# Three PSUM bank pairs kept out of one block's second matmul round, with the output accumulator cleared later

## The chip, the cores and the metric

The kernel runs on one core of one Trainium2 chip. The metric is the device time in microseconds of one launch. Of the kernel before, three runs took 655.49, 655.88 and 656.5 us; the median is 655.88 us.

## What is computed

The reference has three parts, run one after the other on 1152 tokens of 512 features (2 batches of 576 tokens, 8 heads of 64).

1. Attention: for each batch and head, a pooled attention over 144 means of four tokens, repeated four times, plus a local attention in a band of width 7.
2. A layer `g = elu(x @ w_in)`, `y = g @ w_out`, with 2048 hidden features.
3. Four gated experts: `h = max(y @ w1[e], 0)`, `out += p[:, e] * (h @ w2[e])`, with 1024 hidden features each and `p` normalised over the experts.

All is in float32. The kernel splits each matmul operand in two float32r parts, hi and lo, and adds three products (hi hi, hi lo, lo hi), so each product is three matmuls.

## The kernel before, in words

The code is written out engine by engine: each engine has its own list of instructions, and semaphores order them. Nothing is planned by a tool; what stands in the list is the order.

The stages are: the attention of batch 0 alone; four blocks of layer 2 on batch 0, mixed with the attention of batch 1; one block of layer 2 on batch 1 (`group1`); three blocks of layer 2 on the same batch in another form (`block7`, w = 5, 6, 7, called here the first, second and third block); then sixteen steps of the experts (`step2`, `down2`). A block is one slice of 512 hidden features. `block7` and `step2` compute the first product by seven half-size products in place of eight, which are put together by sums on DVE.

A `block7` on TensorE (PE) has two rounds. In the up round it makes seven products for each of two column pairs p = 0, 1, in three pairs of PSUM banks: A = (0, 3), B = (1, 4), C = (2, 5). DVE forms sums over them, ACT takes the exponential of the elu, DVE its maximum (`max_part`) and the lo part (`lo_part`). In the down round (`down(g, f)`) it multiplies the hidden features by `w_out`, in eight groups g = 0 to 7. Each group is 12 matmuls of 288 columns into the bank `DOWN7_BANKS[g]`. Groups 0 to 3 are made in two passes, six matmuls of each and then the other six of each; groups 4 to 7 are made one after the other. DVE adds each finished group to `y_acc` (line 1352) and then runs `beside(g)`, some other work written there:

- first block: `token_sums(g)`, which for g = 0 to 3 makes one of four sums of the other half of the tokens (`add_y`, lines 1432 to 1443);
- second block: `gates(g)`, small operations on the gate;
- third block: `nothing(g)`.

Each addition to `y_acc` raises the semaphore `y_added`. PE waits on it before it writes a bank again. `y_before` is its value when all groups of the block before have been added. In the kernel before, the eight groups of a block have eight different banks, so no group waits for an addition of its own block; the waits stand ahead of the first products of the next block.

Between the second and the third block DVE waits until POOL has made the lo parts of all weight sums (`s_lo_ready`, line 1638), whose raw form lies in the space of `o_acc`, and then sets `o_acc` to zero (line 1553). The third block's DVE work, first `sum_u2` (line 1301), stands behind that. `sum_c22` (line 1311) comes after `sum_u2`, `sum_w`, two `max_part` and two `lo_part`; PE waits for it ahead of the last seven-product pair of bank B (the first matmul of line 572 with `t_hi` and `wa_hi`). POOL makes lo parts of weights and tokens all the while; ACT makes the hi parts.

After the third block DVE forms four sums for the experts (`add_y(1, n)`) and PE goes on with `step2(0, 0)`.

Of the kernel before, what the change touches and what calls it, by code (L numbers as in the profile page):

```python
# [13 lines left out]
BATCH, HEADS, SEQ, HD = 2, 8, 576, 64  # L14
# [29 lines left out]
KC = DM // 128  # L44
FB = 512
FC = FB // 128
BLOCKS1 = D_FF // FB
HALVES2 = D_FF2 // FB
N1 = HALF
T1 = SEQ // N1  # L50
# [4 lines left out]

BLOCKS7 = 3
FIRST7 = 2 * BLOCKS1 - BLOCKS7
DOWN7_BANKS = (6, 7, 0, 3, 1, 4, 2, 5)
XT_COLS = slice(256, 256 + N1)

QF = FB // 2
# [26 lines left out]
OUT_CREDIT, Y_CREDIT, DOWN2_CREDIT, UNIT_CREDIT = 2, len(MOE_BANKS), len(DOWN2_BANKS), PAIRS2  # L88
# [18 lines left out]
def program(nc, q, k, v, w_in, w_out, probs, w1, w2, out):  # L107
# [12 lines left out]
    with ExitStack() as ctx:  # L120
        def sb(name, shape, dt=F32):
            return ctx.enter_context(nc.sbuf_tensor(name, shape, dt))

        def sem(name):
            return ctx.enter_context(nc.semaphore(name))
# [7 lines left out]
        o_acc = sb("o_acc", [128, MT, DM])  # L133
# [82 lines left out]
        def xt_at(t):  # L216

            if t == T3_:
                return slice(None), slice(0, 2), slice(SEQ + N1, 2 * SEQ)
            return slice(None), t, slice(None), XT_COLS  # L220
# [13 lines left out]
        zeros_set, pad_set, acc_zeroed = sem("zeros_set"), sem("pad_set"), sem("acc_zeroed")  # L234
# [10 lines left out]
        s_raw_ready, s_hi_ready, s_lo_ready = sem("s_raw_ready"), sem("s_hi_ready"), sem("s_lo_ready")  # L245
# [15 lines left out]
        y_added = sem("y_added")  # L261
# [25 lines left out]

        GROUPS_LAYER1 = GROUPS1 * BLOCKS1 * BATCH
        UPS_LAYER1 = UP1 * BLOCKS1 * BATCH
        YS_LAYER1 = Y_CREDIT + T1 * KC * BLOCKS1 * BATCH  # L290


        @block.sync
# [82 lines left out]
        def _(pe):  # L376
# [192 lines left out]
            def product2(bank, w_op, x_op, start, stop, done):  # L569

                for k in range(2):
                    nc.tensor.matmul(bank, w_op[0][:, k, :], x_op[0][:, k, :], start=(start and k == 0), stop=False,  # L572
                                     skip_group_check=True)
                    nc.tensor.matmul(bank, w_op[0][:, k, :], x_op[1][:, k, :], start=False, stop=False,  # L574
                                     skip_group_check=True)
                    last = nc.tensor.matmul(bank, w_op[1][:, k, :], x_op[0][:, k, :], start=False, stop=(stop and k == 1),  # L576
                                            skip_group_check=True)
                last.then_inc(done, 1)

            def block7(w):  # L580

                v = w - FIRST7
                t0 = SEQ
                y_before = Y_CREDIT + T1 * KC * w
                h_before = UP1 * w

                def weights(fh, kh, p):
                    at = (slice(None), slice(2 * kh, 2 * kh + 2), slice(QF * fh + 128 * p, QF * fh + 128 * (p + 1)))
                    return wa_hi[at], wa_lo[at]

                def weight_sum(n, p):
                    at = (slice(None), n, slice(None), slice(128 * p, 128 * (p + 1)))
                    return s_hi[at], s_lo[at]

                def tokens(kh, th):
                    at = (slice(None), slice(2 * kh, 2 * kh + 2), slice(t0 + N1 * th, t0 + N1 * (th + 1)))
                    return x_hi[at], x_lo[at]

                def token_sum(n):
                    return t_hi[xt_at(n)], t_lo[xt_at(n)]  # L600

                def bank(banks, p):
                    return psum[:, banks[p], 0:N1]

                pe.wait_ge(wa_lo_ready, KC * w + 2)
                for p in range(PAIRS2):
                    pe.wait_ge(y_added, y_before - 5 + p)
                    product2(bank(BANK_A, p), weights(0, 0, p), tokens(0, 0), True, False, p1_done)
                pe.wait_ge(xt_lo_ready, 1)
                pe.wait_ge(s_lo_ready, 3 * v + 1)  # L610
                for p in range(PAIRS2):
                    pe.wait_ge(y_added, y_before - 3 + p)
                    product2(bank(BANK_B, p), weight_sum(S2, p), token_sum(T2_), True, False, p6_done)
                pe.wait_ge(wa_lo_ready, KC * (w + 1))
                for p in range(PAIRS2):
                    pe.wait_ge(p1_copied, PAIRS2 * v + p + 1)
                    product2(bank(BANK_A, p), weights(0, 1, p), tokens(1, 0), False, True, p2_done)
                pe.wait_ge(xt_lo_ready, 2)
                pe.wait_ge(s_lo_ready, 3 * v + 2)
                for p in range(PAIRS2):  # L620
                    pe.wait_ge(y_added, y_before - 1 + p)
                    product2(bank(BANK_C, p), weight_sum(S1, p), token_sum(T1_), True, False, p5_done)
                pe.wait_ge(xt_lo_ready, 4)
                for p in range(PAIRS2):
                    pe.wait_ge(u2_ready, PAIRS2 * v + p + 1)
                    product2(bank(BANK_B, p), weights(1, 0, p), tokens(0, 1), False, False, p7_done)
                for p in range(PAIRS2):
                    pe.wait_ge(c22_ready, PAIRS2 * v + p + 1)
                    product2(bank(BANK_B, p), weights(1, 1, p), token_sum(T4_), False, True, p4_done)
                pe.wait_ge(s_lo_ready, 3 * v + 3)  # L630
                for p in range(PAIRS2):
                    pe.wait_ge(w_ready, PAIRS2 * v + p + 1)
                    product2(bank(BANK_C, p), weight_sum(S4, p), tokens(1, 1), False, True, p3_done)

                def down(g, f):

                    tt, c = divmod(g, KC)
                    t, cols = slice(t0 + N1 * tt, t0 + N1 * (tt + 1)), slice(128 * c, 128 * (c + 1))
                    to = psum[:, DOWN7_BANKS[g], 0:N1]
                    nc.tensor.matmul(to, wb_hi[:, f, cols], h_hi[:, f, t], start=(f == 0), stop=False)  # L640
                    nc.tensor.matmul(to, wb_hi[:, f, cols], h_lo[:, f, t], start=False, stop=False)  # L641
                    last = nc.tensor.matmul(to, wb_lo[:, f, cols], h_hi[:, f, t], start=False, stop=(f == FC - 1))  # L642
                    if f == FC - 1:
                        last.then_inc(group_done, 1)

                pe.wait_ge(wb_lo_ready, FC * (w + 1))
                pe.wait_ge(h_lo_ready, h_before + 2)
                for g in range(KC):
                    if g >= 2:
                        pe.wait_ge(h_lo_ready, h_before + g + 1)  # L650
                    down(g, 0)
                    down(g, 1)
                for g in range(KC):
                    if g == 0:
                        pe.wait_ge(h_lo_ready, h_before + 5)
                    down(g, 2)
                    if g == 0:
                        pe.wait_ge(h_lo_ready, h_before + 6)
                    down(g, 3)
                pe.wait_ge(h_lo_ready, h_before + 8)  # L660
                for g in range(KC, 2 * KC):
                    for f in range(FC):
                        down(g, f)

            def step2(j, b):
# [26 lines left out]
                    pe.wait_ge(h_lo_ready, UPS_LAYER1 + TILES_STEP * (v - 1) + PAIRS2 * place + p + 1)  # L692

                if isinstance(j, int) and v == 0:
                    pe.wait_ge(y_added, YS_LAYER1 - 4)
                pe.wait_ge(y_lo_ready, Y_PARTS * b + 2)
                pe.wait_ge(wa_lo_ready, KC * w + 2)
                for p in range(PAIRS2):
# [2 lines left out]
                pe.wait_ge(y_lo_ready, Y_PARTS * b + 3)  # L701
                pe.wait_ge(s_lo_ready, 3 * (j + BLOCKS7) + 1)
                for p in range(PAIRS2):
                    pe.wait_ge(y_added, YS_LAYER1 - 3 + p)
                    bank_free(3, p)
                    product2(bank(BANK_B, p), weight_sum(S2, p), token_sum(T2_), True, False, p6_done)
                pe.wait_ge(y_lo_ready, Y_PARTS * b + 6)
# [3 lines left out]
                    product2(bank(BANK_A, p), weights(0, 1, p), tokens(1, 0), False, True, p2_done)  # L711
                pe.wait_ge(s_lo_ready, 3 * (j + BLOCKS7) + 2)
                for p in range(PAIRS2):
                    pe.wait_ge(y_added, YS_LAYER1 - 1 + p)
                    bank_free(2, p)
                    product2(bank(BANK_C, p), weight_sum(S1, p), token_sum(T1_), True, False, p5_done)
                for p in range(PAIRS2):
# [106 lines left out]
            with pe.Fori(FIRST7, 2 * BLOCKS1) as w:  # L824
                block7(w)
# [325 lines left out]
        def _(dve):  # L1151
# [127 lines left out]
            def block7(w, beside):  # L1279
# [68 lines left out]
                for g in range(2 * KC):  # L1348
                    tt, c = divmod(g, KC)
                    at = (slice(None), c, slice(t0 + N1 * tt, t0 + N1 * (tt + 1)))  # L1350
                    dve.wait_ge(group_done, groups_before7(w) + g + 1)
                    nc.vector.tensor_tensor(y_acc[at], psum[:, DOWN7_BANKS[g], 0:N1], y_acc[at], ALU.add).then_inc(y_added, 1)
                    beside(g)
# [195 lines left out]

            block7(FIRST7 + 1, gates)  # L1550

            dve.wait_ge(s_lo_ready, 3 * BLOCKS7)
            nc.vector.memset(o_acc[:], 0.0).then_inc(acc_zeroed, 1)

            def nothing(g):
                pass

            block7(FIRST7 + 2, nothing)
            dve.wait_ge(gate_step, 4)
            for n in range(4):  # L1560
                add_y(1, n)
# [187 lines left out]
```

## Time and profile before

| | |
|---|---|
| median of 3 runs | 655.88 us |
| the profiled execution's own time | 655.88 us |
| its span, first to last instruction | 654.0 us |
| PE busy | 643.4 us (98%) |
| DVE busy | 346.9 us (53%) |
| ACT busy | 287.2 us (44%) |
| POOL busy | 324.4 us (50%) |
| mean granted TensorE clock | 0.999 |

The busy time of PE is that of its matmuls, whose ends are modelled and overlap; the distance from one start to the next is the better measure of its pace. PEld is the load of the weights, which runs beside the matmuls. An engine's idle time costs something only if the engine that sets the end waits for it. A line number in a row is that of the instruction in the listing above; a helper's line serves all its callers.

### The profile page before, as it was taken

What the parts mean: (1) busy time and instruction counts of PE and PEld (TensorE: products, weight loads), DVE (VectorE), ACT (ScalarE), POOL (GpSimd) and SP (SyncE); (2) the same over time, 40 slices, a digit from 0 to 9 for tenths busy, and PEclk for the clock granted to TensorE, in tenths of its full rate; (3) what the DMA queues carried; (4) which work ended last, traced back from release to release, by engine and by line L of the source; (5) the groups of instructions that cost most, each with busy time, mean ns of one, the idle gap of its engine ahead of it and who ended that gap; (6) DMA issues with size and microseconds to landing.
All of it is one profiled execution on the core that took longest, in us unless ns stands there. A gap on an engine that the chain in (4) does not pass through costs nothing.

```text
span 654.0 us, 12954 instructions
## 1 busy us (share of the span) xinstructions
PE 643.4 (98%) x4698; PEld 592.7 (91%) x4698; DVE 346.9 (53%) x758; ACT 287.2 (44%) x778; POOL 324.4 (50%) x282
## 2 busy tenths in 40 slices
PE   8999999999999999999999999999999999999998
PEld 5788999999999999998998898899899899899986
DVE  5856454545456876675544544453464355365342
ACT  4878383838295685564223133142162152142210
POOL 4674444344388799898326237137056065160200
PEclk9999999999999999999999999999999999999999
DMA  9854333322112132301203003002011012010012
GB/s 180 229 140 124 106 99 102 102 70 97 64 66 79 64 117 64 114 15 66 66 1 128 1 0 128 0 29 100 0 64 64 0 64 64 2 64 1 2 49 96
DMA packets 51491, 46.13 MB, mean 71 GB/s; under 512 B 31616, under 2 KB 33920, under 8 KB 51456
## 3 DMA queue, kind: packets, MB, share of 16 engines
q1 hardware_dynamic: 51456, 45.67, 23.6%
q8 instruction: 21, 0.34, 0.2%
q14 instruction: 14, 0.11, 0.1%
HBM read 43.30 MB, written 2.36 MB: 70 GB/s over the span
## 4 chain that ended last, share of the span: by engine, by line
PE 86%; SPq 4%; ACT 4%; DVE 2%; issue 2%; DMA 1%; POOL 0%; ACTq 0%; POOLq 0%; DVEq 0%
PE psum L499 15%; PE psum L500 15%; PE psum L501 15%; PE psum L572 11%; PE psum L576 10%; PE psum L574 10%; SPq L298 2%; PE psum L642 2%; PE psum L641 2%; PE psum L640 2%; DMA k_in<-in_k 1%; SPq L309 1%; ACT attn L852 1%; PE psum L491 1%; DVE neg_max L1188 1%
## 5 line engine op out<-in xcount | busy, mean ns | idle before, releaser
L1597 POOL TENSOR_TENSOR wb_lo<-wb_raw,wb_hi 128x512 fp32r<-128x512 f32 x64 | 81.6, 1292 | 185.5 <-ACT wb_hi L886 185.5
L1412 DVE SCALAR_TENSOR_TENSOR o_acc<-psum,gate_now,o_acc 128x512 f32<-128x512 f32 x72 | 54.1, 751 | 126.0 <-PE psum L501 125.7
L501 PE MATMUL psum<-wb_hi,h_lo 128*128 128x512 f32 x288 | 112.3, 390 | 0.0
L500 PE MATMUL psum<-wb_lo,h_hi 128*128 128x512 f32 x288 | 112.2, 390 | 0.0
L499 PE MATMUL psum<-wb_hi,h_hi 128*128 128x512 f32 x288 | 112.0, 389 | 0.0
L996 ACT ACTIVATE h_hi<-psum 128x320 fp32r<-128x320 f32 (+1 forms) x128 | 52.5, 412 | 87.3 <-DVE psum L1384 40.3
L1597 POOL TENSOR_TENSOR wa_lo<-wa_raw,wa_hi 128x512 fp32r<-128x512 f32 x60 | 77.5, 1316 | 17.4 <-ACT wa_hi L927 17.4
L1002 ACT COPY sums<-psum 128x256 f32<-128x256 f32 (+1 forms) x32 | 12.8, 400 | 155.1 <-PE psum L576 155.1
L576 PE MATMUL psum<-x_hi,wa_lo 128*128 128x256 f32 (+2 forms) x228 | 67.4, 296 | 0.0
L574 PE MATMUL psum<-x_lo,wa_hi 128*128 128x256 f32 (+2 forms) x228 | 67.3, 295 | 0.0
L572 PE MATMUL psum<-x_hi,wa_hi 128*128 128x256 f32 (+2 forms) x228 | 67.3, 295 | 0.0
L501 PEld LDWEIGHTS psum<-wb_hi,h_lo 128*128 128x128 f32 x288 | 54.1, 188 | 11.3
L499 PEld LDWEIGHTS psum<-wb_hi,h_hi 128*128 128x128 f32 x288 | 54.1, 188 | 10.9
L1366 DVE SCALAR_TENSOR_TENSOR h_lo<-psum,h_hi 128x320 fp32r<-128x320 f32 (+1 forms) x128 | 54.8, 450 | 17.1 <-ACT h_hi L996 17.0
L500 PEld LDWEIGHTS psum<-wb_lo,h_hi 128*128 128x128 f32 x288 | 54.0, 188 | 10.8
L499 PE MATMUL psum<-h_hi,wb_hi 128*128 128x288 f32 x160 | 48.5, 303 | 0.0
L501 PE MATMUL psum<-h_hi,wb_lo 128*128 128x288 f32 x160 | 47.1, 294 | 0.0
L500 PE MATMUL psum<-h_lo,wb_hi 128*128 128x288 f32 x160 | 47.1, 294 | 0.0
L574 PE MATMUL psum<-t_lo,s_hi 128*128 128x320 f32 (+2 forms) x152 | 44.9, 295 | 0.0
L576 PE MATMUL psum<-t_hi,s_lo 128*128 128x320 f32 (+2 forms) x152 | 44.8, 295 | 0.0
L572 PE MATMUL psum<-t_hi,s_hi 128*128 128x320 f32 (+2 forms) x152 | 44.8, 295 | 0.0
L572 PEld LDWEIGHTS psum<-x_hi,wa_hi 128*128 128x128 f32 x228 | 43.0, 189 | 0.6
(193 smaller groups left out, 1682.9 us busy)
## 6 DMA issues: line engine op xcount, KB each, us to landing
wa_raw<-in_moe_w_in SPq DMA_DIRECT2D x8, 1024.0 KB, 5.3
wb_raw<-in_moe_w_out SPq DMA_DIRECT2D x8, 1024.0 KB, 5.0
wa_raw<-in_moe_w SPq DMA_DIRECT2D x8, 1024.0 KB, 5.0
wb_raw<-in_moe_w SPq DMA_DIRECT2D x8, 1024.0 KB, 5.0
out<-o_acc SPq DMA_DIRECT2D x9, 256.0 KB, 2.0
q_in<-in_q SPq DMA_DIRECT2D x10, 144.0 KB, 5.0
k_in<-in_k SPq DMA_DIRECT2D x10, 144.0 KB, 4.8
v_in<-in_v SPq DMA_DIRECT2D x5, 288.0 KB
```

The source lines that it names most:

```text
L298: sp.dma_start(dst[:, :, HD * h:HD * (h + 1)], src[:, :, h, :]).then_inc(loaded[held(u)], 16)
L499: nc.tensor.matmul(bank_cols, w_hi(n), x_hi_(n), start=(n == 0), stop=False)
L500: nc.tensor.matmul(bank_cols, w_hi(n), x_lo_(n), start=False, stop=False)
L501: last = nc.tensor.matmul(bank_cols, w_lo(n), x_hi_(n), start=False, stop=(n == chunks - 1))
L572: nc.tensor.matmul(bank, w_op[0][:, k, :], x_op[0][:, k, :], start=(start and k == 0), stop=False, skip_group_check=True)
L574: nc.tensor.matmul(bank, w_op[0][:, k, :], x_op[1][:, k, :], start=False, stop=False, skip_group_check=True)
L576: last = nc.tensor.matmul(bank, w_op[1][:, k, :], x_op[0][:, k, :], start=False, stop=(stop and k == 1), skip_group_check=True)
L640: nc.tensor.matmul(to, wb_hi[:, f, cols], h_hi[:, f, t], start=(f == 0), stop=False)
L996: nc.scalar.activation(h_hi[:, 2 * fh + p, t0 + width * th:t0 + width * (th + 1)], psum[:, bank[p], 0:width], ACT.Relu).then_inc(h_hi_read ...
L1366: nc.vector.scalar_tensor_tensor(h_lo[at], bank(banks, p), 0.0, h_hi[at].bitcast(F32), ALU.max, ALU.subtract).then_inc(h_lo_ready, 1)
L1412: nc.vector.scalar_tensor_tensor(o_acc[:, m, :], psum[:, DOWN2_BANKS[(MT * half + m) % 2], :], gate_now[:, m:m + 1], o_acc[:, m, :], ALU.m ...
L1597: nc.gpsimd.tensor_tensor(lo[:, c, :], raw[:, c, :], hi[:, c, :].bitcast(F32), ALU.subtract).then_inc(lo_ready, 1)
```

## The change

The down groups 4 to 7 of each `block7` no longer use banks 1, 4, 2 and 5. They take banks 6, 7, 6 and 7 again, which groups 0 and 1 used. So PE waits ahead of each of them until the group that last used the bank has been added: group 4 for group 0, 5 for 1, 6 for 4, 7 for 5. Groups 0 and 1 get the wait for the block before, and the up round waits less (only p = 1 of B and C; this is needed after the `group1` block). `step2` loses its four waits on `y_added` inside and gets one. The clearing of `o_acc`, with its wait, moves from between the second and third block to `beside(0)` of the third block, behind the addition of group 0.

```diff
-DOWN7_BANKS = (6, 7, 0, 3, 1, 4, 2, 5)
+DOWN7_BANKS = (6, 7, 0, 3, 6, 7, 6, 7)
...
# block7, product of bank pair B (weight sum S2)
                 for p in range(PAIRS2):
-                    pe.wait_ge(y_added, y_before - 3 + p)
+                    if p == 1:
+                        pe.wait_ge(y_added, y_before - 3)
...
# block7, product of bank pair C (weight sum S1)
                 for p in range(PAIRS2):
-                    pe.wait_ge(y_added, y_before - 1 + p)
+                    if p == 1:
+                        pe.wait_ge(y_added, y_before - 2)
...
# block7, down round
                 for g in range(KC):
-                    if g >= 2:
+                    if g < 2:
+                        pe.wait_ge(y_added, y_before - 1 + g)
+                    else:
                         pe.wait_ge(h_lo_ready, h_before + g + 1)
                     down(g, 0)
                     down(g, 1)
...
                 for g in range(KC, 2 * KC):
+                    pe.wait_ge(y_added, y_before + (1, 2, 5, 6)[g - KC])
                     for f in range(FC):
                         down(g, f)
...
# step2, bank pairs B and C
-                    pe.wait_ge(y_added, YS_LAYER1 - 3 + p)
+                    if p == 1:
+                        pe.wait_ge(y_added, Y_CREDIT + T1 * KC * BLOCKS1 * BATCH)
...
-                    pe.wait_ge(y_added, YS_LAYER1 - 1 + p)
...
# DVE
-            dve.wait_ge(s_lo_ready, 3 * BLOCKS7)
-            nc.vector.memset(o_acc[:], 0.0).then_inc(acc_zeroed, 1)
-
-            def nothing(g):
-                pass
-
-            block7(FIRST7 + 2, nothing)
+            def clear_out(g):
+                if g == 0:
+                    dve.wait_ge(s_lo_ready, 3 * BLOCKS7)
+                    nc.vector.memset(o_acc[:], 0.0).then_inc(acc_zeroed, 1)
+
+            block7(FIRST7 + 2, clear_out)
```

## Rows read from the trace of the kernel before

**Rows 1.** Engines and granted clock, from the page: busy us (share), instructions; then 40 slices.

```profile
PE 643.4 (98%) x4698; PEld 592.7 (91%) x4698; DVE 346.9 (53%) x758; ACT 287.2 (44%) x778; POOL 324.4 (50%) x282
...
PEclk9999999999999999999999999999999999999999
```

**Rows 2.** Busy time by engine in the three blocks: stretch, its length, then each engine.

```profile
core 0: us, PE busy (x) PEld busy (x) DVE busy (x) ACT busy (x) POOL busy (x), PEclk, DMA share, GB/s
202.92:227.02 24.10, 24.10 (x182) 23.87 (x181) 19.80 (x40) 16.99 (x40) 18.66 (x14) 1.00 0.18 58
227.02:251.11 24.09, 24.09 (x183) 23.86 (x181) 15.04 (x38) 17.30 (x41) 23.93 (x20) 1.00 0.28 90
251.11:276.12 25.01, 24.11 (x183) 23.87 (x182) 17.31 (x35) 15.34 (x37) 24.39 (x20) 1.00 0.25 84
```

**Rows 3.** Timeline of PE at the wait for `sum_c22`, blocks one and three: start, duration.

```profile
210.71 0.29 PE L576 MATMUL psum<-x_hi,wa_lo 128*128 128x288 f32 x1
211.00 0.40 PE L572 MATMUL psum<-t_hi,wa_hi 128*128 128x288 f32 x1
211.24 0.29 PE L574 MATMUL psum<-t_lo,wa_hi 128*128 128x288 f32 x1
...
258.89 0.29 PE L576 MATMUL psum<-x_hi,wa_lo 128*128 128x288 f32 x1
260.09 0.40 PE L572 MATMUL psum<-t_hi,wa_hi 128*128 128x288 f32 x1 [0.90 <-DVE psum L1311]
```

**Rows 4.** Timeline of DVE at the same two places (x2: two instructions in one row).

```profile
210.49 1.02 DVE L1311 TENSOR_TENSOR psum<-psum,sums 128x288 f32<-128x288 f32 x2
...
259.58 0.82 DVE L1311 TENSOR_TENSOR psum<-psum,sums 128x288 f32<-128x288 f32 x2
```

**Rows 5.** Timeline of DVE in the first block's down round.

```profile
218.45 0.46 DVE L1352 TENSOR_TENSOR y_acc<-psum,y_acc 128x288 f32<-128x288 f32 x1
...
220.27 0.45 DVE L1352 TENSOR_TENSOR y_acc<-psum,y_acc 128x288 f32<-128x288 f32 x1
...
224.06 1.41 DVE L1443 TENSOR_TENSOR h_spare<-y_acc,h_spare 128x512 f32<-128x512 f32 x1
225.40 1.18 DVE L1352 TENSOR_TENSOR y_acc<-psum,y_acc 128x288 f32<-128x288 f32 x3
```

**Rows 6.** Timeline of PE: groups 4 and 6 begin; the block's last matmul, the next's first.

```profile
220.62 0.29 PE L640 MATMUL psum<-h_hi,wb_hi 128*128 128x288 f32 x1
...
223.82 0.29 PE L640 MATMUL psum<-h_hi,wb_hi 128*128 128x288 f32 x1
...
226.88 0.30 PE L642 MATMUL psum<-h_hi,wb_lo 128*128 128x288 f32 x1
227.02 0.29 PE L572 MATMUL psum<-x_hi,wa_hi 128*128 128x288 f32 x1
```

**Rows 7.** Timeline of DVE, group 0 added: second block, then third block.

```profile
242.53 0.46 DVE L1352 TENSOR_TENSOR y_acc<-psum,y_acc 128x288 f32<-128x288 f32 x1
...
267.54 0.46 DVE L1352 TENSOR_TENSOR y_acc<-psum,y_acc 128x288 f32<-128x288 f32 x1
```

**Rows 8.** Timeline of PE in the third block: first matmul of group 5.

```profile
271.31 0.29 PE L640 MATMUL psum<-h_hi,wb_hi 128*128 128x288 f32 x1
```

**Rows 9.** Timeline of DVE round the clearing of `o_acc`, then of POOL just before it.

```profile
252.91 3.90 DVE L1553 MEMSET o_acc<- 128x4608 f32 x1 [1.14 <-ACT sums L947]
256.72 0.76 DVE L1301 TENSOR_TENSOR sums<-psum,sums 128x288 f32<-128x288 f32 x2
...
249.35 2.53 POOL L1638 TENSOR_TENSOR s_lo<-o_acc,s_hi 128x512 fp32r<-128x512 f32 x2
```

**Rows 10.** One line's instructions: min/median/max ns, first and last start, forms.

```profile
L1436 DVE TENSOR_TENSOR y_acc<-y_acc x2: 826/1123/1420, 220.6 to 277.7; 128x512 f32<-128x512 f32 x1, 128x640 f32<-128x640 f32 x1
```

**Rows 11.** Timeline of PE in step2(0, 1): before and after the waits of bank B.

```profile
287.67 0.31 PE L576 MATMUL psum<-x_hi,wa_lo 128*128 128x320 f32 x1
287.82 0.31 PE L572 MATMUL psum<-t_hi,s_hi 128*128 128x320 f32 x1
```

More of the change, by code:

```diff
@@ L289, in program @@
         UPS_LAYER1 = UP1 * BLOCKS1 * BATCH
-        YS_LAYER1 = Y_CREDIT + T1 * KC * BLOCKS1 * BATCH
         @block.sync
@@ L694, in step2 @@
                 if isinstance(j, int) and v == 0:
-                    pe.wait_ge(y_added, YS_LAYER1 - 4)
+                    pe.wait_ge(y_added, Y_CREDIT + T1 * KC * BLOCKS1 * BATCH - 4)
                 pe.wait_ge(y_lo_ready, Y_PARTS * b + 2)
```

## Prediction

> **What bounds the kernel now.** I read the page first, then the busy time by stretch for the three blocks, then the timelines of PE, DVE and POOL there. PE is busy 98% of the span at full clock, the higher of its two levels, 2.4 GHz [rows 1]. So only what makes PE stand still costs time, and only a stall that goes away gives some back. The reader should see three blocks of 24.10, 24.09 and 25.01 us [rows 2]: the third is 0.91 longer. It is lost in one place, at the wait for `sum_c22`. There the distance between two matmul starts is 210.71 to 211.00, 0.29, in the first block, and 258.89 to 260.09, 1.20, in the third [rows 3], against the usual 0.133. In both PE starts 0.51 after the start of the first `sum_c22` (210.49 to 211.00; 259.58 to 260.09) [rows 3, 4]; I use this 0.51 as the time from the start of a DVE instruction of 288 columns to the matmul that waits for it. After such a stop the next distance is 0.24 in place of 0.133 (211.00 to 211.24) [rows 3]: a stop costs another 0.107.
>
> Why is DVE late in the third block? The clearing of `o_acc` stands between the blocks; the first sum behind it starts at 256.72 [rows 9]. The wait for POOL and the clearing together cost PE those 0.91.
>
> **The change part by part.**
>
> *Freed banks and fewer waits in the up round.* Nothing stands still there now: from the last matmul of a block to the first of the next it is 226.88 to 227.02, 0.14 [rows 6], with a loop's branch and a wait between. A bank that is free earlier gives nothing. The fifteen steps after `step2(0, 0)` lose three waits each. At one of those places the distance is 287.67 to 287.82, 0.15 [rows 11], the pace of 320 columns. So 0; at most the rounding of such a row, 0.01 by 45, -0.45. The block's waits that are met when PE comes to them: four more a block. I take 0 by the 0.14 of rows 6, and as the other end 0.01 for each of twelve, +0.12. PE's next instructions are queued behind each, but the weights and matmuls ahead of it cover it; without the cover the cost would be that 0.107 at each.
>
> *First block, group 6 (the first new stall).* DVE adds each group and then runs one `add_y`. Groups 0 and 1 are added by 218.45 + 0.46 = 218.91 and 220.72 [rows 5]. Group 4 starts on PE at 220.62, group 5 at 222.22 (one group is 12 by 0.133 = 1.60), group 6 at 223.82, the next block at 227.02 [rows 6]. So groups 4 and 5 pass. Group 6 now wants bank 6, so group 4 must have been added. But DVE is behind: the last `add_y` starts at 224.06 and takes 1.41, and the addition of group 4 starts at 225.40, first of three without idle time between [rows 5]. Nothing up to there changes, so the time holds. PE starts group 6 at 225.40 + 0.51 = 225.91, not 223.82: 2.09, and 0.107 behind it, **+2.20**. Group 7 wants group 5, the second of the three in that row, added by 226.3, while PE comes at 227.5: nothing. Queued behind this wait is all of PE's list, so the second block begins 2.20 late. Nothing takes that back: no later wait of PE is set by a DMA or by POOL, whose splits come earlier against PE, which is slack.
>
> *Second block.* Group 4 is added at once when it is done; the gate's operations are short. Nothing: the block stays at 24.09, its `sum_c22` stop included.
>
> *Third block, the stall that goes.* Without the clearing ahead of it the block is as the second: 25.01 to 24.10, **-0.91** [rows 2]. What is late next is the same chain as in the second block, whose 0.29 is in its length.
>
> *Third block, group 5 (the second new stall).* Now the clearing is queued behind the addition of group 0, and the additions of groups 1 to 7 behind it. Group 0's starts 15.51 after the block's begin (242.53 - 227.02) [rows 7, 2]; in the third, less the 0.91, 267.54 - 251.11 - 0.91 = 15.52, the same. DVE begins the next instruction 0.37 later, so the clearing begins at 15.89. Group 5 starts on PE at 271.31 - 251.11 - 0.91 = 19.29 [rows 8, 2] and needs group 1, whose addition is next after the clearing. How long does that hold DVE? From the recorded start to the next instruction it is 256.72 - 252.91 = 3.81 [rows 9]. But the recorded start doesn't fit what it waits for. It waits only for POOL's lo parts, and these end at 249.35 + 2.53 = 251.88 [rows 9]; DVE is free from 252.91 - 1.14 = 251.77; ACT's copy, which the row names, is not in its wait. If the clearing began 0.05 behind POOL (the 0.51 less the 0.46 of an instruction, [rows 4]), at 251.93, it held DVE for 256.72 - 251.93 = 4.79. The two ends are 3.81 and 4.79; I take 4.79, since a wait that is met and an engine that is free leave no other reason for a later start. Then group 1's addition starts at 15.89 + 4.79 = 20.68, PE at 21.19: 1.90 late, and 0.107, **+2.01**. With 3.81 it is 19.70, 20.21, 0.92 and 0.107: +1.03. Groups 1 to 4 are then added 0.37 apart, group 4's starting at 21.8, PE may start group 6 from 22.3 and comes at 22.8: no third stall, with 0.5 to spare. DVE has caught up before the block ends, so the sums for the experts and the new wait in `step2(0, 0)` find what they found.
>
> The Trainium skill has a rule on this price: by "VectorE: DVE Perf Modes", Zero memsets can be issued as uint32 (trn2), a memset takes one cycle per element, and its Specifications give 0.96 GHz. Its estimate is 4608 / 0.96 = 4.80 us, against the recorded 3.90 and my 4.79; by the recorded row the change would cost 2.3, by the rule 3.3.
>
> **Sum.** 2.20 - 0.91 + 2.01 = +3.30 on the profiled execution, whose time is 655.88 with a span of 654.0, 1.88 around it. This time equals the median of the three runs, so no correction: **659.2 us**.
>
> **The rivals.**
>
> *A, the record is right about the clearing (3.81).* For it: it is the row. Against: the idle 1.14 ahead of it has no reason. 2.20 - 0.91 + 1.03 = +2.3: 658.2.
>
> *B, no first stall.* The first stall hangs on DVE's backlog, which comes from `add_y` taking 1.42 for 512 columns while POOL works, where 640 columns take 0.83 later [rows 10]. At that rate 512 take 0.66, DVE would be done with all four before 223.3, and group 6 would pass. 655.88 - 0.91 + 2.01 = 657.0. Against: nothing ahead of it is changed. By the Trainium skill, "SBUF — State Buffer", Who interferes with whom, a DVE instruction with two SBUF inputs and a POOL instruction that reads SBUF exclude each other and the order of issue decides; the trace shows the longer times, and by that rule a small shift of POOL could change them.
>
> *C, faster: PE is bound by no addition.* Place: groups 5 and 6. The mechanism would be that DVE is ahead of PE in its queue in the down rounds, so that the additions are done when PE comes and only the clearing's removal from between the blocks is felt: -0.91, 655.0. It decides from the point where group 4's addition starts before 223.82 - 0.51 = 223.31 in the first block, and group 1's before 19.29 - 0.51 = 18.78 in the third. The rows have 225.40 and, at the best, 19.70. For it speaks only that DVE is 53% busy over the span.
>
> *D, the clearing is over early.* Were it to run at twice the recorded speed in its new place, 1.9, group 1 would be added in time: 2.20 - 0.91 = +1.3: 657.2.
>
> *E, a stall more.* If additions after the clearing are slower than 0.37 apart, group 6 of the third block stands too; and after stops of 2 us PE might lose clock. The clock is at its upper level in all 40 slices [rows 1], so no row shows such a loss. From +4: 659.9 and more.
>
> **How the numbers follow.** Forecast 0.62, A 0.17, B 0.06, C 0.05, D 0.05, E 0.05. The range should hold the forecast and A: from 658.2 less 0.5 (the spread of the runs, 655.49 to 656.50, is about 0.5 either side) and the 0.45 of the waits in part, 657.5, to 659.2 plus 0.5 and a little of E, 660.2. A measurement here tells 0.2%, 1.3 us, from no change. Slower by more: the forecast, A, E: 0.84. C's 0.9 is less than that, so it counts as faster only with a little gained besides: 0.03 of its 0.05. Within: B, D and the rest of C, 0.13.
>
> **What would show it.** In the profile after: the first block about 26.3 long, with one distance near 2.2 ahead of group 6's first matmul, released by an addition to `y_acc` (line 1352's); the second block 24.1; the third about 26.1, with a `sum_c22` distance of 0.29 and one near 2.0 ahead of group 5. The clearing beginning by the record about 1 us after the addition of group 0 has let go of DVE would show that the record is late, and 4.79 right. From the first matmul of `step2(0, 0)` to the end nothing changes. The forecast is wrong if PE starts group 6 of the first block without a stop, or if another of the groups 4 to 7 stands still.

## The result

The changed kernel takes 660.55 us (median of 4 runs, 659.74 to 661.26) against 656.00 for the kernel before (4 runs), a ratio of 1.0069 with a 95% interval of 1.0051 to 1.0087: 4.5 us slower. The forecast was 3.3 slower than the 655.88 it started from, 659.2, with a range up to 660.2; the measured time lies above it.

The title counts three bank pairs and one block. By the code it is two pairs, B and C, that no down group uses any more, in each of the three blocks; pair A still takes groups 2 and 3.

The page of the changed kernel, its span, PE's busy time and the granted clock in 40 slices, beside [rows 1]:

```profile
span 658.5 us, 12934 instructions
...
PE 645.4 (98%) x4698; PEld 594.3 (90%) x4698; DVE 346.1 (53%) x758; ACT 286.8 (44%) x778; POOL 323.9 (49%) x282
...
PEclk9999999999999899999999999999999999999999
```

The three blocks, to be read against [rows 2]:

```profile
core 0: us, PE busy (x) PEld busy (x) DVE busy (x) ACT busy (x) POOL busy (x), PEclk, DMA share, GB/s
202.70:230.45 27.75, 25.86 (x183) 25.40 (x181) 19.86 (x40) 16.98 (x40) 22.30 (x17) 0.94 0.23 80
230.45:254.55 24.10, 24.10 (x183) 23.87 (x181) 15.40 (x38) 17.30 (x41) 20.71 (x17) 1.00 0.17 61
254.55:280.60 26.05, 24.35 (x182) 23.89 (x181) 17.43 (x35) 15.22 (x37) 24.14 (x20) 1.00 0.31 106
```

They last 27.75, 24.10 and 26.05 us, where they lasted 24.10, 24.09 and 25.01: 4.70 more in all. The stretch before them, in which the kernels' work is the same, is 0.22 shorter (the first block begins at 202.70, not 202.92). It varies from execution to execution (in the profile of run 1 below the first block begins at 203.46). That leaves 4.5, the growth of the span from 654.0 to 658.5. So all that is lost is lost here. The mean clock in the first block is 0.94: that is the part I had not counted.

The first block's group 6 on PE, beside [rows 6]: the matmul before it, the two after the stop, and then the pace, in which the distances can be read from the starts.

```profile
223.45 0.29 PE L643 MATMUL psum<-h_hi,wb_lo 128*128 128x288 f32 x1
225.64 0.40 PE L641 MATMUL psum<-h_hi,wb_hi 128*128 128x288 f32 x1 [1.89 <-DVE y_acc L1356]
225.88 0.29 PE L642 MATMUL psum<-h_lo,wb_hi 128*128 128x288 f32 x1
...
226.14 0.44 PE L641 MATMUL psum<-h_hi,wb_hi 128*128 128x288 f32 x1
226.38 0.44 PE L642 MATMUL psum<-h_lo,wb_hi 128*128 128x288 f32 x1
226.62 0.44 PE L643 MATMUL psum<-h_hi,wb_lo 128*128 128x288 f32 x1
```

```profile
229.50 0.31 PE L643 MATMUL psum<-h_hi,wb_lo 128*128 128x288 f32 x1
229.65 0.29 PE L641 MATMUL psum<-h_hi,wb_hi 128*128 128x288 f32 x1
229.78 0.29 PE L642 MATMUL psum<-h_lo,wb_hi 128*128 128x288 f32 x1
```

PE stops for 225.64 - 223.45 = 2.19, which is 2.06 over the pace, and the next distance is 0.24, as forecast. But from 226.14 to 229.50 each distance is 0.24 in place of 0.133: 14 distances, 14 by 0.107 = 1.50 us. The granted clock of that stretch is a half, the lower level of 1.2 GHz; from the block's begin to the stop no two starts on PE were more than 0.3 apart:

```profile
core 0: us, PE busy (x), PEclk, DMA share, GB/s
226.14:229.50 3.36, 3.36 (x16) 0.50 0.50 134
```

DVE at the same place, beside [rows 5], and its clearing of `o_acc` in the third block with the additions behind it, beside [rows 7, 9]:

```profile
223.82 1.39 DVE L1447 TENSOR_TENSOR h_spare<-y_acc,h_spare 128x512 f32<-128x512 f32 x1
225.14 0.81 DVE L1356 TENSOR_TENSOR y_acc<-psum,y_acc 128x288 f32<-128x288 f32 x2
```

```profile
270.07 0.46 DVE L1356 TENSOR_TENSOR y_acc<-psum,y_acc 128x288 f32<-128x288 f32 x1
271.44 3.90 DVE L1559 MEMSET o_acc<- 128x4608 f32 x1 [0.91 <-issue]
275.25 1.12 DVE L1356 TENSOR_TENSOR y_acc<-psum,y_acc 128x288 f32<-128x288 f32 x3
```

PE in the third block, at the wait for `sum_c22` beside [rows 3], and at group 5 beside [rows 8]:

```profile
262.33 0.29 PE L575 MATMUL psum<-x_hi,wa_lo 128*128 128x288 f32 x1
262.62 0.40 PE L571 MATMUL psum<-t_hi,wa_hi 128*128 128x288 f32 x1
...
273.71 0.29 PE L643 MATMUL psum<-h_hi,wb_lo 128*128 128x288 f32 x1
275.70 0.40 PE L641 MATMUL psum<-h_hi,wb_hi 128*128 128x288 f32 x1 [1.70 <-DVE y_acc L1356]
```

The last `add_y` of the first block holds DVE until 225.14, and group 6 starts 0.50 later. At `sum_c22` the distance is 262.62 - 262.33 = 0.29, where it was 1.20. In the third block the addition of group 0 starts at 270.07 and lets go of DVE 0.37 later, at 270.44; the clearing is recorded from 271.44, and the addition of group 1 starts at 275.25. DVE is thus held for 4.81, with 0.9 of it ahead of the record's start, in which nothing is waited for ("issue"). The stop at group 5 is 275.70 - 273.71 = 1.99, or 1.86 over the pace.

| term | forecast | measured |
|---|---|---|
| first block, group 6, stop and restart | +2.20 | 2.06 + 0.11 = +2.17 |
| lower clock behind it | 0 | +1.50 |
| third block, `sum_c22` | -0.91 | -0.91 |
| third block, group 5, stop and restart | +2.01 | 1.86 + 0.11 = +1.97 |
| sum | +3.30 | +4.73 |

### The profile page after: what moved, and what is told of

It reads as the page before. It is cut to its first block, busy times and chain, and to the rows that moved or that the text cites. A ratio compares the mean times of both kernels' runs of the same rounds, so it can differ in the third digit from the quotient of the medians.

```text
span 658.5 us, 12934 instructions
## 1 busy us (share of the span) xinstructions
PE 645.4 (98%) x4698; PEld 594.3 (90%) x4698; DVE 346.1 (53%) x758; ACT 286.8 (44%) x778; POOL 323.9 (49%) x282
## 4 chain that ended last, share of the span: by engine, by line
PE 86%; SPq 4%; ACT 4%; DVE 3%; DMA 1%; issue 1%; POOL 0%; ACTq 0%; POOLq 0%
PE psum L498 15%; PE psum L500 15%; PE psum L499 15%; PE psum L571 11%; PE psum L573 11%; PE psum L575 11%; SPq L297 2%; PE psum L641 2%; PE psum L643 2%; PE psum L642 2%; DMA k_in<-in_k 1%; SPq L308 1%; SPq L305 1%; ACT attn L856 1%; PE psum L490 1%
```

## The experiments

All times are medians; the kernel before took 656.01 beside the first four, 656.37 beside the next four and 656.37 beside the last three. The range in brackets behind a ratio means the 95% interval of the ratio to it. The profile shows one execution of each run; of the others the mean clock and the time are known.

**1. The old banks, the clearing moved.** Only the DVE part of the change:

```diff
 DOWN7_BANKS = (6, 7, 0, 3, 1, 4, 2, 5)      # and all waits of before
...
+            def clear_out(g):
+                if g == 0:
+                    dve.wait_ge(s_lo_ready, 3 * BLOCKS7)
+                    nc.vector.memset(o_acc[:], 0.0).then_inc(acc_zeroed, 1)
+
+            block7(FIRST7 + 2, clear_out)
...                                         # the clearing between the blocks goes
```

> The eight banks and all waits of the kernel before, only the clearing of o_acc moved behind the first addition of the third block. My theory (the loss is made by groups 5 and 6 waiting for additions that stand in DVE's queue behind other work, and by the lower clock after the first stop): no stop at a down group, the third block 24.1 long in place of 25.0, time 656.0 - 0.9 = 655.1. Rival (the moved clearing itself costs, wherever the groups' banks are): third block above 25.0, time above 656.0.

655.37 us, ratio 0.9987 (0.9978 to 0.9996). DVE in its third block, as in the changed kernel:

```profile
267.18 0.46 DVE L1352 TENSOR_TENSOR y_acc<-psum,y_acc 128x288 f32<-128x288 f32 x1
268.55 3.90 DVE L1555 MEMSET o_acc<- 128x4608 f32 x1 [0.91 <-issue]
272.37 1.85 DVE L1352 TENSOR_TENSOR y_acc<-psum,y_acc 128x288 f32<-128x288 f32 x5
```

DVE is just as late: group 1 is added at 272.37, and four more behind it in one go. PE had begun group 5 at 270.95, without a stop, since the groups have banks of their own:

```profile
270.82 0.30 PE L642 MATMUL psum<-h_hi,wb_lo 128*128 128x288 f32 x1
270.95 0.29 PE L640 MATMUL psum<-h_hi,wb_hi 128*128 128x288 f32 x1
```

The third block is 24.10 long (251.65 to 275.75), as expected. The gain is 0.64 by the medians, less than the 0.91 of the rows but with the 0.91 inside the interval (0.3 to 1.4). The late addition costs nothing by itself; the bank taken again turns it into a stop.

**2. The new banks, the clearing back between the blocks.**

```diff
-                if g == 0:      # in clear_out(g)
-                    dve.wait_ge(s_lo_ready, 3 * BLOCKS7)
-                    nc.vector.memset(o_acc[:], 0.0).then_inc(acc_zeroed, 1)
+            dve.wait_ge(s_lo_ready, 3 * BLOCKS7)
+            nc.vector.memset(o_acc[:], 0.0).then_inc(acc_zeroed, 1)
```

> The changed kernel with the clearing of o_acc back between the second and third block. Theory: the stop of 2.06 ahead of group 6 of the first block stays, with 0.11 behind it and, if the clock falls because of this stop, about 1.5 more; no stop ahead of group 5 in the third block, its sum_c22 distance 1.20 again. 656.0 + 2.2 + 1.5 = 659.7; without the fall of the clock 658.2. Rival (the lower clock comes from the later stop or from the moved clearing): 658.2 in all executions.

658.31 us, ratio 1.0040 (1.0026 to 1.0054). The only stops of its blocks are these two:

```profile
226.36 0.40 PE L641 MATMUL psum<-h_hi,wb_hi 128*128 128x288 f32 x1 [1.88 <-DVE y_acc L1356]
```

```profile
261.54 0.29 PE L575 MATMUL psum<-x_hi,wa_lo 128*128 128x288 f32 x1
262.51 0.40 PE L571 MATMUL psum<-t_hi,wa_hi 128*128 128x288 f32 x1 [0.67 <-DVE psum L1315]
```

The first stop is there and group 5 of the third block passes. Five executions split in two sorts: three with a mean clock of 0.999 or 1.0 take 658.27 to 658.31, two with 0.997 and 0.996 take 659.38 and 658.98. So the clock can fall without the second stop and without the moved clearing, and it doesn't fall always. The profiled execution is one without a fall, so this run doesn't show where it falls in the two others; in the changed kernel's profile it is behind the first stop, and run 3, which lacks that stop, has no fall. My 659.7 took the fall for certain. The `sum_c22` distance is 0.97, not 1.20: PE comes 2.2 later, and POOL, for which the clearing waits there, is done earlier against it. POOL's lo parts end at 254.05, before the last addition lets go of DVE at 254.33 (its start 253.96 and 0.37); in the kernel before they ended 0.2 after it. The first stop gave that 0.23 back. From 254.33 to the first sum at 259.14 the clearing holds DVE for 4.81.

**3. The new banks, the clearing moved, the token sums behind groups 4 to 7.**

```diff
-                if g < 4:
-                    add_y(0, g)
+                if g >= 4:
+                    add_y(0, g - 4)
```

> The changed kernel with the four token sums of the first block behind groups 4 to 7 in place of 0 to 3. Theory: group 4 is added as soon as it is done, group 6 doesn't stand, and the clock stays at its upper level in the first block; left is the stop of 1.86 at group 5 of the third block: 656.0 + 1.96 - 0.91 = 657.05. Rival (the clock falls at this place by the new waits, not by the stop): 1.5 more, 658.5.

657.29 us, ratio 1.0016 (1.0006 to 1.0025). No stop at a down group of the first block, no fall of the clock in 11 executions (0.999 or 1.0). What is left is one row:

```profile
272.80 0.40 PE L641 MATMUL psum<-h_hi,wb_hi 128*128 128x288 f32 x1 [1.71 <-DVE y_acc L1356]
```

With the reuse of banks in place, one change in DVE's order takes both the first stop and the clock's loss away.

**4 and 5. The clearing in nine pieces of 512 columns, on top of run 3.** First with two pieces behind group 7:

```diff
-                    nc.vector.memset(o_acc[:], 0.0).then_inc(acc_zeroed, 1)
+                for m in ((g,) if g < 7 else (7, 8)):
+                    nc.vector.memset(o_acc[:, m, :], 0.0).then_inc(acc_zeroed, 1)
...
-            dve.wait_ge(acc_zeroed, 1)
+            dve.wait_ge(acc_zeroed, MT)
```

> As the run with the sums behind groups 4 to 7, and the clearing in nine pieces of 512 columns, one behind each of groups 0 to 6 and two behind group 7. Theory: neither stop, both gains: all three blocks 24.1, time 655.1, although the banks are reused as in the changed kernel. Rival (bank reuse costs by itself, by ordering PE behind DVE, or the pieces cost DVE more than one clearing): above 656.

656.24 us, ratio 1.0004 (0.9995 to 1.0013). Both stops are gone, yet the gain is too: in the second step of the experts PE waits for POOL.

```profile
288.99 0.31 PE L575 MATMUL psum<-t_hi,s_lo 128*128 128x320 f32 x1
289.88 0.41 PE L571 MATMUL psum<-x_hi,wa_hi 128*128 128x320 f32 x1 [0.58 <-POOL x_lo L1617]
```

That is 0.74 over the pace of 0.147. DVE makes the sums for the experts behind group 7, ACT and POOL split them. With two pieces ahead, the first of these sums starts at 277.33, against 276.54 in the next run, and about as much came through to PE. My expectation overlooked who stands behind group 7. The next run only places the pieces otherwise:

```diff
-                for m in ((g,) if g < 7 else (7, 8)):
+                for m in ((0,), (1,), (2,), (3,), (4, 5), (6, 7), (8,), ())[g]:
```

> The run with late sums and the clearing in nine pieces, but placed one behind each of groups 0 to 3, two behind 4 and 5, one behind 6 and none behind 7. Theory: the stop of 0.74 of the run before, in the second step of the experts, where PE waited for POOL's lo part of the tokens, came of the two pieces behind group 7, which put DVE's sums for the experts late; it goes, and the time is that of the run with old banks, 655.4, with the banks reused. Rival (the pieces cost by their number): stays near 656.2.

655.47 us, ratio 0.9983 (0.9974 to 0.9992): 0.9 us less than the kernel before, and less than the changed one, with banks 1, 4, 2 and 5 still free of down groups. Run 1 gained 0.64 with the old banks. So the gain is that of the clearing's new place; the banks, once DVE is in time, cost nothing and give nothing that these runs show. Its DVE:

```profile
267.20 0.46 DVE L1356 TENSOR_TENSOR y_acc<-psum,y_acc 128x288 f32<-128x288 f32 x1
267.71 0.48 DVE L1560 MEMSET o_acc<- 128x512 f32 x1
268.12 0.40 DVE L1356 TENSOR_TENSOR y_acc<-psum,y_acc 128x288 f32<-128x288 f32 x1
...
272.77 0.46 DVE L1356 TENSOR_TENSOR y_acc<-psum,y_acc 128x288 f32<-128x288 f32 x1
273.29 1.03 DVE L1560 MEMSET o_acc<- 128x512 f32 x2
274.38 0.46 DVE L1356 TENSOR_TENSOR y_acc<-psum,y_acc 128x288 f32<-128x288 f32 x1
```

Each addition comes before PE wants the bank.

**6. A shorter first stop.** The fourth token sum behind group 4:

```diff
-                if g < 4:
-                    add_y(0, g)
+                if g in (0, 1, 2, 4):
+                    add_y(0, min(g, 3))
```

> The changed kernel with the fourth token sum of the first block behind group 4 in place of group 3, so that group 4 is added about 1.3 earlier. Theory (the stop ahead of group 6 is the backlog of DVE, and a stop of about 2 in this place lets the clock fall in some executions): the stop is 0.6 to 0.8 in place of 2.06, no fall of the clock in any execution: the 657.3 of the run with late sums plus 0.8 = 658.1. Rival (a stop of any length here lets the clock fall): mean clock 0.997 in some executions and those above 659.

658.33 us, ratio 1.0034 (1.0022 to 1.0046).

```profile
224.82 0.40 PE L641 MATMUL psum<-h_hi,wb_hi 128*128 128x288 f32 x1 [0.59 <-DVE y_acc L1356]
```

The stop is 0.75 over the pace: what DVE has ahead of group 4's addition sets it. The clock is 0.999 or 1.0 in all 6 executions.

**7. A stop of 2.1 in the third block.** On top of run 3:

```diff
                 if g == 0:
                     dve.wait_ge(s_lo_ready, 3 * BLOCKS7)
+                    nc.vector.memset(o_acc[:, 0, 0:128], 0.0).then_inc(acc_zeroed, 1)
+                    dve.wait_ge(acc_zeroed, 1)
                     nc.vector.memset(o_acc[:], 0.0).then_inc(acc_zeroed, 1)
...
-            dve.wait_ge(acc_zeroed, 1)
+            dve.wait_ge(acc_zeroed, 2)
```

> The run with late token sums (no stop in the first block), and a clearing of 128 columns more ahead of the clearing of o_acc, so that the stop at group 5 of the third block grows from 1.86 to about 2.1, as long as the first block's stop was. Theory L (the length of the stop decides whether the clock falls): in some executions a mean clock of 0.997 and a time near 658.8, the others near 657.6. Rival P (the first block's place decides): clock 1.0 in all, 657.6.

657.53 us, ratio 1.0019 (1.0010 to 1.0029). The stop is 2.12 over the pace. In one execution of 11, the profiled one, the clock fell here (0.997, 658.26):

```profile
272.05 0.40 PE L641 MATMUL psum<-h_hi,wb_hi 128*128 128x288 f32 x1 [1.97 <-DVE y_acc L1356]
...
273.67 0.44 PE L643 MATMUL psum<-h_hi,wb_lo 128*128 128x288 f32 x1
273.91 0.44 PE L641 MATMUL psum<-h_hi,wb_hi 128*128 128x288 f32 x1
```

The others took 656.93 to 657.84. So the place in the first block is not needed. Why only one execution in 11 has a fall here, and more had one with the first block's stop, these runs don't show.

**8. A stop of 6.8 there.** Also on top of run 3, the clearing twice, with the same wait between.

```diff
                 if g == 0:
                     dve.wait_ge(s_lo_ready, 3 * BLOCKS7)
                     nc.vector.memset(o_acc[:], 0.0).then_inc(acc_zeroed, 1)
+                    dve.wait_ge(acc_zeroed, 1)
+                    nc.vector.memset(o_acc[:], 0.0).then_inc(acc_zeroed, 1)
...
-            dve.wait_ge(acc_zeroed, 1)
+            dve.wait_ge(acc_zeroed, 2)
```

> The run with late token sums, with the clearing of o_acc made twice, so that the stop at group 5 of the third block is about 6.8 in place of 1.86. Both theories on the hold of a clearing: if one holds DVE 4.8 the time grows by 4.9 over 657.3, to 662.2; if 3.9, to 661.2. Theory L (length): the clock falls in all executions, 1.5 more, 663.7 in all. Rival P (place): the clock stays, 662.2.

664.48 us, ratio 1.0125 (1.0109 to 1.0140), the clock at 0.992 to 0.995 in all 4 executions.

```profile
267.18 0.46 DVE L1356 TENSOR_TENSOR y_acc<-psum,y_acc 128x288 f32<-128x288 f32 x1
268.55 3.90 DVE L1559 MEMSET o_acc<- 128x4608 f32 x1 [0.91 <-issue]
273.48 3.90 DVE L1561 MEMSET o_acc<- 128x4608 f32 x1 [1.03 <-issue]
277.29 1.49 DVE L1356 TENSOR_TENSOR y_acc<-psum,y_acc 128x288 f32<-128x288 f32 x4
```

```profile
277.74 0.61 PE L641 MATMUL psum<-h_hi,wb_hi 128*128 128x288 f32 x1 [6.63 <-DVE y_acc L1356]
278.15 0.44 PE L642 MATMUL psum<-h_lo,wb_hi 128*128 128x288 f32 x1
```

From one clearing's record to the next it is 4.93, and the stop grew by 6.79 - 1.86 = 4.93: with about 0.1 for the wait between, the clearing holds DVE 4.8, not 3.9. Behind the stop the distances are about 0.24 until 282.95: from the restart to the block's last matmul it is 7.11, against 4.78 in run 3, 2.33 more. 657.29 + 4.93 + 2.33 = 664.55, measured 664.48; I had counted 1.5 for the clock.

**9 to 11. Where the clock falls.** The changed kernel again; a stop of 1.8 in the first block (a clearing of 1080 bfloat16 columns of an unused tensor in the place of the fourth sum, which goes behind group 4); and a stop of 2.9 there (a clearing of 900 columns behind the fourth sum). The last two, in short:

```diff
# run 10
-                if g < 4:
-                    add_y(0, g)
+                if g in (0, 1, 2, 4):
+                    add_y(0, min(g, 3))
+                if g == 3:
+                    nc.vector.memset(filler[:], 1.0)
...
# run 11
+        filler = sb("filler", [128, 900], BF16)
...
                 if g < 4:
                     add_y(0, g)
+                if g == 3:
+                    nc.vector.memset(filler[:], 1.0)
```

> The changed kernel once more, for more executions. Theory: those with a mean clock of 1.0 take about 659.5, those with 0.997 about 1 to 1.5 more; the stops are the same in both.

660.29 us, ratio 1.0061 (1.0047 to 1.0074). Four of five executions had 0.997 and took 660.12 to 660.90; the one with 1.0 took 659.58. A fall goes with 0.5 to 1.3 more, somewhat less than I had expected. In the profiled execution (0.997) the stops are 2.06 and 1.87; that they are the same without a fall is not shown here.

> The run with the short stop in the first block, with a clearing of 1080 columns of an unused tensor in the place of the fourth token sum, so that the stop ahead of group 6 is about 1.9, as long as the third block's, which never let the clock fall. Theory L (length decides): clock 1.0 in all executions, 658.3 + 1.2 = 659.5. Rival P (the place in the first block decides): 0.997 in some executions, as with 2.04.

659.36 us, ratio 1.0049 (1.0036 to 1.0063). The clock is 0.999 or 1.0 in all 5 executions; the first stop is 1.82 over the pace:

```profile
225.37 0.41 PE L642 MATMUL psum<-h_hi,wb_hi 128*128 128x288 f32 x1 [1.67 <-DVE y_acc L1357]
```

> The changed kernel with a clearing of 900 columns of an unused tensor behind the fourth token sum, so that the stop ahead of group 6 is about 3.0 in place of 2.06. Theory L: the clock falls in all executions; 1.0 more stop on the time of the changed kernel's executions with a fall, about 661.5 to 662. Rival (chance alone, whatever the length): falls in some only.

661.23 us, ratio 1.0080 (1.0065 to 1.0096); the clock 0.997 in all 4 executions.

```profile
226.48 0.61 PE L642 MATMUL psum<-h_hi,wb_hi 128*128 128x288 f32 x1 [2.79 <-DVE y_acc L1357]
226.88 0.44 PE L643 MATMUL psum<-h_lo,wb_hi 128*128 128x288 f32 x1
227.12 0.44 PE L644 MATMUL psum<-h_hi,wb_lo 128*128 128x288 f32 x1
```

Here the pace is 0.24 from the restart on. The time is 0.3 under what I had expected, and 0.9 of stop over run 9 brought 0.94.

A clock at half its level for 3.4 us lowers the mean of 659 us by 0.0026. So I count a mean of 0.997 or less as a fall. The profiles agree: each with such a mean shows the slow stretch, and none with 0.999 or 1.0 does.

| longest stop in the three blocks (in the profile), over the pace | runs | executions with a fall (mean clock 0.997 or less) |
|---|---|---|
| 1.86 or 1.87 | 3, 6, 10 | 0 of 22 |
| 2.04 to 2.12 | changed kernel, 2, 7, 9 | 11 of 26 |
| 2.95 | 11 | 4 of 4 |
| 6.79 | 8 | 4 of 4 |

In these runs the length of the stop goes with the fall, in either place. Between 2.04 and 2.12 some executions have it and some don't. By the Trainium skill, "TensorE: Matmul & The Clock Gate", What's actually happening, the clock is set by how busy PE has been recently. The table agrees in that the longer stops have the more falls.

## Why the prediction was wrong

**Where the time is lost** was right: only in the three blocks, at groups 6 and 5, and nowhere in the up rounds or the steps, where fewer waits gave nothing and more waits cost nothing (the second block is 24.10 against 24.09).

**The first new stop** was right in place, releaser and size: 2.17 against 2.20. Runs 3 and 6 show the cause, DVE's order: without the fourth sum ahead of group 4's addition the stop is 0.75, without the four there is none. Rival B, no stop there because the sums run faster, did not come; the last of them took 1.39.

**The stall that goes** was right, 0.91, and the third block's `sum_c22` distance is back at 0.29.

**The second new stop** was right, 1.97 against 2.01, and with it the reading that the clearing holds DVE for 4.79 and not for the 3.81 that its record shows. Rival A would have made 1.03. Run 8, where a second clearing and a wait added 4.93 to the stop, bears it out. The estimate from the rule of the Trainium skill that the prediction cites ("VectorE: DVE Perf Modes", 4.80) agrees with the 4.81.

**The step that failed** is the one that put no term for the clock between the first stop and the sum. I wrote that the clock stays at its upper level in all 40 slices, so that no row shows a loss, and gave "after stops of 2 us PE might lose clock" a share of a rival of 0.05. But the longest idle time on PE in the three blocks of the kernel before is 0.90, so its even clock told nothing of a stop of 2. The lower clock is worth 1.50 in the profiled execution, and 1.43 is what the sum lacks (4.73 against 3.30). That a stop of this length brings the fall is shown by the table: 11 of 26 executions at 2.04 to 2.12, none of 22 at 1.87 or less. Executions without a fall took 659.74 and 659.58, 0.4 to 0.5 over the forecast and inside the range; those with a fall took 660.1 to 661.3.

**No change or faster** (rivals C and D): no row of the changed kernel speaks for them. What C wanted to be true is true of run 5, where the additions are ahead of PE: that kernel, with the banks reused, is 0.9 faster than before.

## What to carry to other kernels

A buffer taken again earlier ties its writer to everything that stands ahead of the release in the releasing engine's queue: look there for the longest instruction, and put it behind the release that is wanted first. In a kernel whose matmul engine never rests, a stop may cost more than its length, since the clock may fall behind it (here 1.5 on top of 2.1); where a change makes such a stop and the kernel before has none as long, the clock needs a term with a chance of its own. And a long instruction's hold is best read from the instructions on both sides of it.

## What the runs showed of the hardware

A clearing of 4608 float32 columns on DVE is recorded with 3.90 us and holds the engine for 4.81 (270.44 to 275.25) and, twice in a row, 4.93 apart. Most of the idle time ahead of its record, 0.91 to 1.03, belongs to it. Read the same way in run 5, one piece of 512 columns, recorded with 0.48, holds DVE for 0.55 (267.57 to 268.12), and two hold it for 1.24 (273.14 to 274.38).

After a stop of 2.06 the clock fell 0.5 us after PE had begun again (in the changed kernel's profile) and stayed low for 3.4; in runs 7 and 9 it fell some 1.4 and 1.2 after; after stops of 2.95 and 6.79 the pace was low from the restart on. The cause of the different shares of executions in the middle row of the table (8 of 10 for the changed kernel, 2 of 5 and 1 of 11 for runs 2 and 7) stays open. One difference is on record: the changed kernel has a second stop, of 1.86, in the third block, and runs 2 and 7 have none of that length besides their first. In both profiles of the changed kernel the fall came before that second stop. Runs 2, 7 and 9 also ran on different chips. No run tells whether either of the two matters.
